# GpSimd sends the rows of inverses out on its own queue, and the first two W_outs are loaded later

## The reference, cut to what matters

```python
# q, k, v: 2 batches x 8 heads x 768 positions x 64
scores = 0.125 * q @ k^T + bias            # bias: -slope of the head * distance
scores = where(keep, scores, -1e9)         # keep: 8 global keys, or 0 <= i - j < 96
a = exp(scores - max);  a = a / (sum(a) + 1e-9)
x = (a @ v) as [1536 tokens, 512]
h = x @ w_in1;  g = h * sigmoid(h);              x = g @ w_out1     # 512 -> 2048 -> 512
h = x @ w_in2;  g = h * clip(h + 3, 0, 6) / 6;   out = g @ w_out2
```

## Time and profile before

| | us |
|---|---|
| median of 3 runs | 581.17 (581.11 to 582.68) |
| the profiled execution's own time | 582.91 |
| its span, first to last instruction | 581.0 |
| TensorE busy | 572.3 (99%) |
| VectorE, ScalarE, GpSimd busy | 369.5, 329.0, 260.9 |
| mean granted clock of TensorE | 0.997 |

### The profile page before, as it was taken

One profiled execution on the slowest core, in us unless ns is written; L12 is line 12 of the kernel. 1 busy time (PEld: TensorE's weight loads), 2 busy tenths in 40 slices (PEclk: granted clock), 3 DMA queues, 4 the chain that ended last, 5 costly groups with the idle time before them and its releaser, 6 DMA issues.

```text
span 581.0 us, 9616 instructions
## 1 busy us (share of the span) xinstructions
PE 572.3 (99%) x3438; PEld 517.9 (89%) x3438; DVE 369.5 (64%) x682; ACT 329.0 (57%) x639; POOL 260.9 (45%) x258
## 2 busy tenths in 40 slices
PE   8979999999999999999999999999999999999998
PEld 6758899999999999999999999999998999999996
DVE  7868898667544867576555686575459675555331
ACT  7858876454444665444555666454556664555441
POOL 6546757669333036295333317494331344331110
PEclk9989999999999999999999999999999999999999
DMA  6778421422221013213212203212111243111002
GB/s 237 251 293 266 148 101 67 144 73 74 73 73 64 28 55 110 72 38 96 59 64 74 72 9 138 72 44 87 54 70 37 74 157 132 56 55 37 1 2 108
DMA packets 16995, 53.25 MB, mean 92 GB/s; under 512 B 2130, under 2 KB 2738, under 8 KB 16946
## 3 DMA queue, kind: packets, MB, share of 16 engines
q1 hardware_dynamic: 16514, 51.83, 26.6%
q10 hardware_dynamic: 432, 0.79, 0.4%
HBM read 49.41 MB, written 3.19 MB: 91 GB/s over the span
## 4 chain that ended last, share of the span: by engine, by line
PE 93%; DMA 3%; ACT 1%; DVE 1%; SPq 1%; issue 0%; POOL 0%; DVEq 0%; POOLq 0%
PE ps L1177 40%; PE ps L1268 23%; PE ps L1259 15%; PE ps L1260 8%; PE ps L1149 2%; DMA inv_rows<-turned 2%; PE ps L1127 2%; PE ps L1103 2%; ACT probs L875 1%; DMA inverses<-inv_rows 1%; SPq L290 0%; DVE negs L642 0%; PE ps L1135 0%; SPq L231 0%; DMA words<-in_counts 0%
## 5 line engine op out<-in xcount | busy, mean ns | idle before, releaser
L428 POOL TENSOR_TENSOR wo_lo<-wo_raw,wo_hi 128x1024 fp32r<-128x1024 f32 x32 | 76.8, 2399 | 237.2 <-ACT wo_hi L935 237.2
L1177 PE MATMUL ps<-x_hi,wi_hi 128*128 128x384 f32 x448 | 150.3, 335 | 0.0
L1177 PE MATMUL ps<-x_lo,wi_hi 128*128 128x384 f32 x448 | 149.9, 335 | 0.0
L1177 PE MATMUL ps<-x_hi,wi_lo 128*128 128x384 f32 x448 | 149.8, 334 | 0.0
L618 DVE TENSOR_TENSOR c_sb<-ps,p_c 128x384 f32<-128x384 f32 x64 | 35.7, 557 | 151.5 <-PE ps L1177 151.4
L915 ACT ACTIVATE p_c<-ps 128x384 f32<-128x384 f32 x64 | 31.5, 492 | 121.5 <-PE ps L1177 121.5
L1177 PEld LDWEIGHTS ps<-x_hi,wi_hi 128*128 128x128 f32 x448 | 84.1, 188 | 1.7 <-issue 0.3
L1177 PEld LDWEIGHTS ps<-x_hi,wi_lo 128*128 128x128 f32 x448 | 84.1, 188 | 0.5
L1177 PEld LDWEIGHTS ps<-x_lo,wi_hi 128*128 128x128 f32 x448 | 84.1, 188 | 0.0
L1020 ACT ACTIVATE g_hi<-g_f 128x768 fp32r<-128x768 f32 x64 | 50.6, 839 | 46.3 <-DVE g_f L628 25.9
L1268 PE MATMUL ps<-wo_hi,g_lo 128*128 128x512 f32 (+1 forms) x194 | 75.3, 388 | 0.0
(11 more groups left out here) (112 smaller groups left out, 1043.3 us busy)
## 6 DMA issues: line engine op xcount, KB each, us to landing
wi_raw<-in_w_in SPq DMA_DIRECT2D x32, 512.0 KB, 3.4
wo_raw<-in_w_out SPq DMA_DIRECT2D x32, 512.0 KB, 3.3
v_raw<-in_v SPq DMA_DIRECT2D x8, 704.0 KB, 4.9
k_raw<-in_kT SPq DMA_DIRECT2D x7, 464.0 KB, 5.0
inverses<-inv_rows SPq DMA_DIRECT2D x24, 128.0 KB, 3.0
out_y<-y_out SPq DMA_DIRECT2D x11, 256.0 KB, 5.3
q_raw<-in_qT SPq DMA_DIRECT2D x6, 384.0 KB, 5.9
q_raw<-in_qT ACTq DMA_DIRECT2D x1, 384.0 KB, 4.6
```

The source lines that it names most:

```text
L428: nc.gpsimd.tensor_tensor(wo_lo[:, s % 2, :], wo_raw[:, s % 2, :], wo_hi[:, s % 2, :], ALU.subtract).then_inc(wo_lo_ok, 1)
L1177: mm = nc.tensor.matmul(p_bank(bank), w[:, s % 2, at], x[:, b, k, :], start=fresh and k == 0 and i == 0, stop=k == 1 and i == 2, skip_grou ...
```

## The change

SyncE no longer issues `rows_out`; GpSimd does, in front of `total(2k+4)` for k = 0 to 9, then k = 10 behind the last total and k = 11 behind the four sums of x for the last two products. The load of the first W_out moves from behind `rows_in(1)` to behind `rows_in(3)`, that of the second to behind `rows_in(6)`, and `wo_high(0)` on ScalarE moves from round 5 to round 6. The load of the second W_in stays.

```diff
+WI_AT = {1: (1,)}
+WO_AT = {3: (0,), 6: (1,)}
...
-                def rows_out(m):
-                    sp.wait_ge(turned_kept, m + 1)
-                    sp.dma_start(inv_rows[m].rearrange("h (u q) -> (h u) q", q=P), turned[:, :]).then_inc(inv_out, 16)
...
                 for m in range(NM):
-                    rows_out(m)
                     if m in QK_AT:
                         next_qk(QK_AT[m])
                     rows_in(m)
                     if m in V_AT:
                         next_v(V_AT[m])
-                    if m == 1:
-                        load_wi(sp, 1)
-                        load_wo(sp, 0)
-                        load_wo(sp, 1)
+                    for s in WI_AT.get(m, ()):
+                        load_wi(sp, s)
+                    for s in WO_AT.get(m, ()):
+                        load_wo(sp, s)
...
+            def rows_out(m):
+
+                pool.wait_ge(turned_kept, m + 1)
+                pool.dma_start(inv_rows[m].rearrange("h (u q) -> (h u) q", q=P), turned[:, :]).then_inc(inv_out, 16)
...
+                    if r >= 4 and r % 2 == 0:
+                        rows_out(r // 2 - 2)
                     total(r)
...
+                rows_out(NM - 2)
                 for n in (2, 3):
                     for half in range(2):
                         x_sum(0, n, half)
+                rows_out(NM - 1)
...
-                    if m == 5:
+                    if m == 6:
                         wo_high(0)
```

## The result

The changed kernel takes 586.45 us (median of 4 runs, 585.01 to 587.86), the kernel before beside it 581.20 (4 runs). The ratio on record is 1.0069, with a 95% interval of 1.0048 to 1.0091, which is 2.8 to 5.3 us; the quotient of the two medians is 1.0090, which is 5.25 us. It is slower by more than the noise, though by less than 1%, where 576.4 was forecast and 580.5 was the end of the range.

A forecast was written before the change was run, and what follows sets the result against it. TensorE, 99% busy, was taken to lose time only where rows go through DRAM. Gains of 3.76 + 1.64 + 0.3 = 5.7, less 0.7 for late writes and 0.2 for wo_high(0), gave 581.17 - 4.8 = 576.4 us, range 575.0 to 580.5.

The forecast's parts named there:

- Round 5 gives all of its 3.76 back: Attention round 5: both edits remove VectorE's 3.54 us wait for the rows' write, so its whole 3.76 us excess goes.
- Round 6 gives its 1.64: Attention round 6: without TensorE's 3 us gap in front, the granted clock returns to 1.00, a gain of 1.64 us.
- Round 3 gives 0.3: Attention round 3: 0.3 of its 0.67 us excess is gained, as copy_rows(1) also waited for a write there.
- SyncE gains too: SyncE, no longer held at rows_out(0), issues k and q 1.5 us sooner; no term in the sum.
- The issue on GpSimd costs c = 1.0: Issuing one rows DMA holds GpSimd 1.0 us, between bounds of 0.3 and 1.57, twelve times.
- The answer time A = 2.4: From GpSimd reaching the write's instruction until SyncE and VectorE see it done: 2.4 us, between 1.23 and 4.13.
- The margins: Slack for the writes behind GpSimd's preparations: 2.3, 2.5 and 2.2 us at the tightest, 2.5 to 4 in other rounds.
- late ones: Writes k = 6, 7 and 11 overrun their margins by 0.1, 0.1 and 0.2 us; taken as 0.7 with scatter.
- totals late, seen as VectorE's inverses waiting for GpSimd: Sign that the forecast is wrong: GpSimd's totals come late and VectorE's inverses wait for them.
- The slower one: Rival: GpSimd answers late every round, each copy_rows waiting through single-buffered turned; +2.5 us, 583.7, chance 0.17.
- the engines are shared: Rival: the 4 KB write waits for loads on any queue, only the moved megabyte helps; gain 2.3, 578.9, chance 0.12.
- The two rules: GpSimd DMAs: 2-port VectorE copies block descriptors, none in these rounds; fixed cost about 2.0 us would make the sum -5.2.

The follow-up runs named there:

- e1: The kernel before with only the two W_outs and wo_high(0) moved, SyncE still issuing the rows; 582.60 us against 581.33 before.
- e15: The changed kernel with GpSimd's issue of the rows one piece of preparation earlier for k up to 4 only; 585.43 us against 581.85 before.
- e5: The changed kernel with each rows_out one piece of preparation earlier on GpSimd, right behind total(2k+3); 581.44 us against 581.88 before.
- e17: The changed kernel with two buffers for the rows, used in turn; 586.32 us against 582.12 before.
- e3: The changed kernel with ScalarE issuing the rows on its own queue, behind the first exponentials of each round; 581.64 us against 581.33 before.

## Why the prediction was wrong, point by point

**Round 5 gives all of its 3.76 back: half.** It gave 1.84. Taking 1024 KB out does it, as e1 shows (5.70), and the write on GpSimd undid a half: issued at 28.04, 1.5 us behind the ready rows, it took 5.99 us (in e1 4.37 us, issued at once). The text said that it "no longer stands behind v, W_in, k and q". It stands behind all four; only the queue had changed.

**Round 6 gives its 1.64: nothing.** In the profile the granted clock is 0.76 again. The term was also not one of the median: in 56 of 103 runs of the kernel before the mean clock is 1.000, and those have nothing to give back. The profiled execution lay 1.7 us above the median, and the text took "the difference, not the level, over"; but this term was that difference, so it stood in the sum although the median run didn't have it. "No gap of 3 us" was the wrong condition: in the changed kernel TensorE idled 1.69 us in round 5 and 2.25 in round 8, and the stretches at 1.2 GHz came behind both. Round 3 idled 2.13 and none came, so the rows do not show what decides it. In e15's profile rounds 6 and 9 take 8.00 and 8.36 us at a clock of 1.000.

**Round 3 gives 0.3: it lost 1.93.** SyncE no longer waits at rows_out(0), so k and q of the third pair went out at 14.08 instead of 15.60, in front of the write, which took 5.9 us from 15.45 instead of 4.13. The prediction named this under "SyncE gains too". It is the sign that was wrong: the queue's owner, once free, sends its loads sooner.

**The issue on GpSimd costs c = 1.0: less.** 0.575 us in the median, 0.740 at most, inside the bounds of 0.3 and 1.57. It was not the cause: e5 has the same 0.57 and no loss.

**The answer time A = 2.4: the step that failed.** Measured from issue to landing it is 3.6 us in the median and 4.8 to 6.0 for k = 0, 2, 4, 5 and 6, the writes that meet loads. It is 4.2 and 3.1 for k = 8 and 9, with v on the engines, 2.4 to 2.5 for k = 1, 3 and 7, and 1.9 and 1.6 for k = 10 and 11, with nothing on them. It was built up from 1.23 us on an emptier queue with 0.5 for busy engines. The 4.13 of the earlier trace rows was a row for a write among loads, and the argument "most of that was queue" put it away: on the shared engines a queue of loads and one's own queue were alike. It was not the longest without a W_out ahead either: SyncE issued rows_out(3) at 35.59 and saw it done at 39.96, 4.37 us.

The margins were priced in the wrong rounds. Of the three "late ones", k = 7 and 11 were answered in 2.5 and 1.6 us, and for k = 6, with 4.8, VectorE waited 0.3 us. What lost was k = 0, 2, 5 and 8: VectorE waited 2.9, 1.9 and 1.6 us for the first three, and the write of k = 8, issued 2.4 us late behind a low part of x, stands in the chain with 4.21. These were among "the other rounds", with 2.5 to 4. The late cost, put at 0.7, is mostly what rounds 8, 9 and 11 lost, 5.1 us, of which 1.6 is the slow clock of round 9.

e5 splits the error of 10 us in two. With every issue at once behind the rows, its writes take 4.1 us in the median and it is level with before: the forecast gain of 4.8 is gone. How much of that is the answer time, and how much is excess that no order of these issues gives back, is not separated. The place behind GpSimd's preparations costs the other 5. The sign "totals late, seen as VectorE's inverses waiting for GpSimd" did not come: that wait is 0.3 us in both profiles.

**The rivals.** The slower one, with A = 4.1 and 583.7 us and a break-even at 3.8, was nearest in time and in mechanism, and got 0.17. It was wrong in one point: the single buffer does not carry the loss (e17). The other rival, "the engines are shared", was right as a mechanism too, and was priced alone: it forecast a gain of 2.3 because it left GpSimd's lateness out. What happened is both together: the write waits for the loads on any queue, and its late issue puts more of them ahead.

**The two rules.** The fixed cost of about 2.0 us that the Trainium skill (DMA: Bandwidth & Descriptors, "Anatomy of one DMA — SWDGE (gpsimd) path") gives fits the free engines: the landings there are 1.9 and 1.6 us. As a price for this kernel it was off by a factor of two and more for the writes among loads, since what ruled was not the fixed part. The rule on 2-port copies had no case here, and no run shows it.
On queues that share the engines the trace of the changed kernel shows rows_out(5) with its first packet at 52.66, behind v (until 51.6) and nearly all of k (until 52.8), though issued at 48.74. The Trainium skill (DMA: Bandwidth & Descriptors, "Queues, rings and completion order") has each engine turn between its queues after a group of descriptors, typically 9 to 17. v has 128 packets, 8 for each of 16 engines if they are evenly spread; by the lower end of that figure the write would have come right behind v, an estimate, and the trace has it about 1 us later. With the upper end a part of k would go ahead too, as it did. The records don't name the engine of a packet, so this stays open.

## What to carry to other kernels

Price a small DMA by the nearest row for one that met the same load on the engines, not by one from an empty queue: here 4 KB on a queue of its own still waited for the megabytes sent before it. So count what is issued ahead on all queues, and for a step that is moved also what its old engine will now send sooner. And when the work sits in a round trip without slack (here rows, DRAM, inverses, the bank, the next turn), put its issue right at the event that it waits for: one piece of preparation in front of it was worth 5 us of 581, a second buffer nothing. Before an excess of a profiled execution is put into a sum on the median, look whether the median run has it: here the mean granted clock of each run would have told.

## What the runs showed of the hardware that was not expected

- A 4 KB write on a queue of its own started its first packet 3.0 to 3.9 us after the issue when 0.7 to 2 MB of loads had just been issued on another queue, and 1.1 us after it on free engines. The same write of SyncE or ScalarE started 0.75 to 0.77 us after the issue on free engines (before, k = 10 and 11; e3, k = 10 and 11).
- GpSimd is held 0.53 to 0.74 us by issuing one 4 KB DMA; SyncE is for 0.30.
- Cutting loads in two or four did not let the small write through sooner (median 4.4 us against 3.6).
- One kernel's repeats differ by up to 6 us here (before: 578.70 to 584.76 over 28 runs), and its profiles differ in which round holds the stall. The number of stretches at the lower clock differs too: mean clocks of 1.000, 0.997 and 0.994 in 56, 35 and 9 of 103 runs, with medians of 581.3, 582.7 and 583.7 us. A single profile told where time can be lost, and only the medians told how much.
